# A two-expert routing step moved up in a fused attention, expert and feed-forward kernel: one product sooner, with the second expert's tokens turned inside the first's last product

## What is computed

```python
# 1 attention with sinks and a window (B=2, H=8, S=768, D=64; 4 sinks, window 128)
scores = scale * q @ k.T;  keep = is_sink | (0 <= rel < window)
a = softmax(where(keep, scores, -1e9));  x = a @ v          # -> 1536 tokens x 512

# 2 eight experts, each takes exactly cap = 1536 // 8 = 192 tokens
logits = x @ w_gate
for idx in argsort(-logits.flatten()):                       # greedy, best pair first
    tok, e = idx // E, idx % E
    if assigned[tok] >= 0 or counts[e] >= cap: continue
    assigned[tok] = e;  counts[e] += 1
out[mask_e] = relu(x[mask_e] @ w1[e]) @ w2[e]                # 512 -> 1024 -> 512

# 3 feed-forward: h = x @ w_in (512 -> 2048);  g = max(h,0) + alpha*min(h,0);  g @ w_out
```

## Time and profile before

| | us |
|---|---|
| median of 3 runs | 631.12 |
| lowest, highest | 629.16, 631.72 |
| the profiled execution | 630.74 |
| its span from first to last instruction | 628.9 |
| TensorE busy / its weight loads busy | 609.8 / 555.8 |
| VectorE / ScalarE / GpSimd busy | 415.6 / 309.1 / 199.2 |

### The profile page before, as it was taken

How to read it: one execution, slowest core, us unless ns; L and a number is a source line. 1 busy time by engine, 2 the same in 40 slices (tenths; PEclk the granted TensorE clock), 3 DMA queues, 4 the chain that set the end, 5 groups by cost and what they waited for, 6 DMA issues and landing times.

```text
span 628.9 us, 12910 instructions
## 1 busy us (share of the span) xinstructions
PE 609.8 (97%) x4932; PEld 555.8 (88%) x4932; DVE 415.6 (66%) x1155; ACT 309.1 (49%) x718; POOL 199.2 (32%) x213
## 2 busy tenths in 40 slices
PE   7899999899999999999999999999999999999996
PEld 4699988669899989899988998999988999999995
DVE  8689998887396978843959787448677520035552
ACT  5888876311123665432246554222556542346663
POOL 5899871010121343120123431301233410123231
PEclk9999999799999999999999999999999999999999
DMA  7478845553630261037003500460017610000001
GB/s 263 152 268 273 304 164 183 205 176 119 224 122 1 91 207 49 0 133 261 2 2 118 210 18 2 171 223 1 2 68 276 233 61 1 1 1 1 2 0 50
DMA packets 31380, 72.89 MB, mean 116 GB/s; under 512 B 2900, under 2 KB 2968, under 8 KB 31320
## 3 DMA queue, kind: packets, MB, share of 16 engines
q1 hardware_dynamic: 27392, 61.22, 28.0%
q0 software_dynamic: 1984, 6.29, 3.0%
q10 hardware_dynamic: 1944, 4.56, 2.0%
HBM read 65.74 MB, written 6.33 MB: 115 GB/s over the span
## 4 chain that ended last, share of the span: by engine, by line
PE 88%; DVE 6%; POOL 2%; issue 2%; DMA 1%; ACT 1%; POOLq 0%; DVEq 0%
PE bank L1724 21%; PE bank L1709 21%; PE bank L1619 14%; PE bank L1610 13%; PE bank L1501 3%; PE bank L1345 3%; PE bank L1403 3%; PE bank L1365 3%; PE bank L1426 2%; DMA rank_row<-key_row 1%; PE bank L1567 1%; PE bank L1588 1%; PE bank L1320 1%; POOL k_lo L390 1%; PE bank L1385 1%
## 5 line engine op out<-in xcount | busy, mean ns | idle before, releaser
L655 POOL TENSOR_TENSOR wi_lo<-w_in,wi_hi 128x512 fp32r<-128x512 f32 x64 | 90.4, 1414 | 271.5 <-ACT wi_hi L813 271.5
L1051 DVE TENSOR_SCALAR beats<-rank_row,key 128x512 bf16<-128x512 f32 (+11 forms) x144 | 90.6, 655 | 11.5 <-PE bank L1503 11.5
L1724 PE MATMUL bank<-wo_lo,g_hi 128*128 128x512 f32 x192 | 75.9, 395 | 0.9 <-DVE wo_lo L1286 0.9
L1724 PE MATMUL bank<-wo_hi,g_hi 128*128 128x512 f32 x192 | 75.7, 394 | 0.0
L1724 PE MATMUL bank<-wo_hi,g_lo 128*128 128x512 f32 x192 | 75.6, 394 | 0.0
L1302 DVE SCALAR_TENSOR_TENSOR g<-bank,g_neg 128x384 f32<-128x384 f32 x64 | 35.4, 553 | 50.5 <-ACT g_neg L865 50.4
L863 ACT ACTIVATE g_neg<-bank 128x384 f32<-128x384 f32 x64 | 31.4, 491 | 66.1 <-PE bank L1709 65.2
L1292 DVE TENSOR_TENSOR g_lo<-g,g_hi 128x384 fp32r<-128x384 f32 x64 | 46.5, 726 | 19.5 <-ACT g_hi L870 19.1
L839 ACT ACTIVATE h_t<-bank 128x192 f32<-128x192 f32 x64 | 21.1, 330 | 73.5 <-PE bank L1610 71.6
L1709 PE MATMUL bank<-y_hi,wi_hi 128*128 128x384 f32 x256 | 56.7, 343 | 0.0
L1709 PE MATMUL bank<-y_lo,wi_hi 128*128 128x384 f32 x256 | 55.2, 336 | 0.0
(11 more groups left out here) (195 smaller groups left out, 1352.0 us busy)
## 6 DMA issues: line engine op xcount, KB each, us to landing
w_a<-moe_w SPq DMA_DIRECT2D x8, 1024.0 KB, 5.2
w_a<-moe_w SPq DMA_DIRECT2D x4, 2048.0 KB, 10.4
w_b<-moe_w SPq DMA_DIRECT2D x8, 1024.0 KB, 5.3
w_b<-moe_w SPq DMA_DIRECT2D x4, 2048.0 KB, 10.2
k_raw<-k_t SPq DMA_DIRECT2D x11, 512.0 KB, 5.8
q_raw<-q_t SPq DMA_DIRECT2D x11, 512.0 KB, 4.7
w_in<-moe_w_in SPq DMA_DIRECT2D x8, 512.0 KB, 5.8
w_out<-moe_w_out SPq DMA_DIRECT2D x8, 512.0 KB, 5.4
```

The costliest lines, as they stand in the source:

```text
L655: nc.gpsimd.tensor_tensor(out=wi_lo[:, f % 2, :, :], in0=w_in[:, :, f * P:(f + 1) * P], in1=wi_hi[:, f % 2, :, :].bitcast(F32), op=ALU.sub ...
L1051: return nc.vector.tensor_scalar(out=beats[:, c % 3, lo:hi], in0=rank_row[:, lo:hi], scalar1=key[:, c:c + 1], scalar2=None, op0=op)
L1724: last = nc.tensor.matmul(DOWN_BANK[t][:, :], a[:, f % 3, t * P:(t + 1) * P], w[:, f % 2, :], start=(f == 0 and n == 0), stop=(f == FC - 1 ...
```

## The change

During expert 0, round 1's last column (11) is counted behind product 6 instead of 7, the maximum across partitions behind 7 instead of 8, the sums behind product 8's start (done 8) instead of its middle (8.5), and the picks in the middle of product 9 instead of behind it. The second expert's tokens are turned in the middle of product 11 (done 11.5) and not between the experts; the four clock-keeping products that stood ahead of the turning are dropped. On ScalarE, `copy_x(1)` moves ahead of the last y_hi copy of expert 0 and so ahead of `load_row(2)`, as it stood already in the later groups.

```diff
             def expert(r):
 
                 j, e = r // 2, r % 2
-                if r < 2:
+                if r == 0:
                     copy_x(r)
...
                     nc.scalar.copy(y_hi[:, m, e * CAP:(e + 1) * CAP], M_BANK[m % 2][:, 0:CAP]).then_inc(y_hi_done, 1)
-                    if r in (2, 4, 6) and m == 2:
-                        copy_x(r + 1)
                     if r == 0 and m == 2:
                         store_keys(2)
+                    if e == 0 and m == 2:
+                        copy_x(r + 1)
                 if r == 0:
                     load_row(2)
...
-            SECOND_ROUND = {1: (3,), 2: (4,), 3: (5, 6), 4: (7,), 5: (8,), 6: (9, 10), 7: (11,)}
+            SECOND_ROUND = {1: (3,), 2: (4,), 3: (5, 6), 4: (7,), 5: (8,), 6: (9, 10, 11)}
...
+                    if done == 7:
+                        across(1)
                     if done == 8:
-                        across(1)
-                    if done == 8.5:
                         before_and_loads(1)
-                    if done == 10:
+                    if done == 9.5:
                         pick_tokens(1)
                     if done == 11:
                         turn_keys(2)
+                    if done == 11.5:
+                        turn_tokens(1)
...
-                if j == 0:
-                    keep_clock(4, DOWN_BANK[2])
-                    turn_tokens(1)
                 for k in range(NM):
                     product(2 * j + 1, k)
```

## The result

The changed kernel took 634.25 us in the median of 5 runs (633.11 to 635.08) against 631.12 us before, also of 5 runs (629.16 to 631.72): **3.1 us slower, ratio 1.0052 [1.0038, 1.0065]**. Two more sets of runs of the same kernel, beside the experiments, gave 1.0042 [1.0027, 1.0056] and 1.0062 [1.0043, 1.0081]. The profiled execution took 635.08 us with a span of 632.3 us.

A forecast was written before the change was run, and what follows sets the result against it. TensorE was taken to bound the kernel, with 88% of the chain of waits; a first count 3.5 us later, the saved 1.65 us becoming waiting time, plus 1.75 us of lowered clock gave +5.25 us: 636.3 us, range 629.4 to 638.4.

The forecast's parts named there:

- the largest term: Round 2's row load, queued behind all of w2_b, delays the first count from 174.82 to 178.3: +3.5 us (3.0 to 3.9).
- The second expert sooner: TensorE after product 11: the second expert starts at 167.01 instead of 168.66, 1.65 us sooner.
- The two shifts of the issues: ScalarE issues the row load 0.93 us later, at 167.22; SyncE issues its two weight loads 1.31 us earlier.
- The row's landing: The row load begins when w2_b is nearly through and lands at 177.0 (176.3 to 177.4), about 1.7 us behind w2_b.
- a line: Loads of SyncE's and ScalarE's queues are set up in order of issue, so the row waits for w2_b, issued ahead.
- The gap: TensorE finishes the second expert's four products at 172.2 and stands still 6.1 us before the first count.
- The clock: The idle gap lowers TensorE's clock to 0.50 for some 3.5 us, losing 1.75 us (0.85 to 3.4).
- The sum: Later first count 3.5 plus lowered clock 1.75 makes +5.25 us over the whole kernel, giving 636.3 us.
- The rival of the shared queues: No line at the row load: it lands at 172.2, first count 1.2 us sooner, 629.9 us; chance 0.25.
- same 7.17 us: The row load takes 7.17 us as before from its later issue, first count +0.93 us, 632.0 us; chance 0.12.

The follow-up runs named there:

- e9: Changed kernel with row load right behind the keys' store, w2_b held until expert 1's tokens are turned, w1_b's second half not waiting for gathers: 630.58 us, 1.0000.
- e10: Changed kernel with row load right behind the keys' store, w2_b and w1_b's second half both held until the second expert's tokens are turned: 628.81 us, 0.9973.

## Why the prediction was right, and where it was not

The direction and the place were right, and the time lay in the range: 636.3 forecast, 634.25 measured. Of the mechanism, the later issue of the row, the wait and the lowered clock were right; the largest term, a row that stands behind all of w2_b, was not. The prediction named its own test for that, "I am wrong if the row's packets start before w2_b's last ones", and they did: about 300 of w2_b's 1024 packets had moved. By its steps, from the turning of the keys:

- **The second expert sooner.** Forecast 1.65 us, measured 5.29 - 3.59 = 1.70 us. The copies of x_gt and the turning cost nothing more, and the moved routing pieces found their inputs ready.
- **The two shifts of the issues.** Row later by 0.93 us: from the keys' turning, 2.92 us before and 3.80 us after, so 0.88. w2_b sooner by 1.31 us: 3.04 and 1.72, so 1.32.
- **The row's landing, the step that failed.** I had the row begin when w2_b was nearly through, and land at 177.0, 9.8 us after its issue. It began 3.5 to 3.6 us after its issue and took 7.3 to 8.0 us, against 3.7 and 7.2 before. So w2_b ahead of it cost the row 0.1 to 0.8 us against the kernel before, where I had 2.6, and no later start. That there is a line was right for the w1_b half; that the row stands behind all of a load issued before it was not. My evidence, 414 packets ahead of the row before, could not tell a part from a whole, since a whole half of w1_b is that size. The term was forecast at +3.5 us on the first count and measured +1.0 to +1.7 (12.43, 13.00 and 13.12 us from the keys' turning in the three profiles, against 11.45). On average that is 1.4 us: 0.88 from the row's later issue and 0.5 from its longer way.
- **The gap.** Forecast 6.1 us, measured 3.4 to 4.1, for the same reason.
- **The clock.** Forecast 1.75 us lost, measured 1.74 us by filling the gap. That the two agree to 0.01 us is luck: I had put it at 0.85 to 3.4, and the measurement is no closer than 0.7 to 3.5. The low stretch was 6.8 us in one of the three profiles of the change and 3.4 in the others. The granted clock fell already with half the gap that I had reckoned with.
- **The sum.** The measured terms, about 1.4 and 1.74, make the 3.1 us. My 5.25 is too much by the line alone. The sign did not hang on that term: the later issue and the clock alone make the kernel slower.

The rival of the shared queues (629.9) had its part: once both have packets they take turns, and the row passes most of w2_b. The rule that it came from, in the Trainium skill, DMA: Bandwidth & Descriptors, Queues, rings and completion order, is the packet-by-packet turn of an engine between the queues that have work. The runs agree with it from the row's first packet on and not before that: no packet of the row moves for 3.5 us after its issue in the changed kernel, against 1.0 to 1.5 us with nothing ahead. The rival "same 7.17 us" (632.0), to which I gave 0.12, was nearest in the row's start and in its landing, and missed the clock; with the measured 1.74 us for that it would have said 633.8.

What I did not settle is where the line is. The counts would fit a place ahead of the engines' queues where the loads of SyncE and ScalarE are turned into packets in the order of issue, a piece at a time. That is a guess: no view here shows that place, and no run varies the size of w2_b.

## What to carry to other kernels

Before moving work earlier, list the DMAs that its results release, and write down their order against every other load of the other queue: here 1.3 us won for a 2 MB load that nobody waited for put it ahead of a 768 KB load that everybody waited for, which was itself issued 0.9 us later. Issue the load that is needed first, and hold a bulk load with a wait on a semaphore at hand. Held until the row's issue, w2_b was late for nothing and the wait was worth some 5 us against the change; held until the row had landed, it was late for its own product. Where TensorE must wait for some microseconds, count the wait and the low clock behind it; products of zeros in the gap bring back the second.

## What the runs showed of the hardware that I had not expected

- **The clock in the light stretch at the end of the first round differs from execution to execution.** In the earlier trace rows it is at 0.50 for all of 117.4 to 127.7. In the changed kernel's first profile it was low only here, and 1.00 behind it:

```profile
116.95:120.36 3.41, 3.41 (x65) 3.41 (x64) 3.41 (x11) 3.41 (x6) 0.00 (x0) 0.50 0.83 312
120.40:127.70 7.30, 6.14 (x79) 3.56 (x77) 5.55 (x29) 1.30 (x3) 0.00 (x0) 1.00 0.02 5
```

  The same kernel's second profile had 10.2 us at 0.50 there, and reached the keys' turning 0.93 us later (163.27 against 162.34). I take the low clock for the cause, which no run isolates. Such differences are a part of the scatter of 2 to 3.5 us between executions of one kernel, and the reason to measure inside a profile from a common event.
- **How small a gap is followed by a low clock.** 1.69 us idle was, in one execution; 1.58 (at the turning in e9), 1.15, 1.10, 0.77 and 0.49 us were not, in one each.
- **A gather beside a bulk load** took 6.18 us instead of 3.4 us, although the two gathers of an expert move 0.39 MB together. The wait that kept SyncE's half off the gathers earned its place: without it the kernel took 1.8 us more than with the half held (e9 and e10, side by side).
